# Other SBUF addresses for the tiles of an attention and two-layer MLP kernel

## The chip, the cores and the metric

The kernel runs on one core of a Trainium2 chip. The metric is the device time of one execution in microseconds (us). TensorE is called PE here, VectorE DVE, ScalarE ACT, GpSimd POOL, and the DMA queue of SyncE SP.

## The reference, cut to what matters

Gated linear attention over 4 batches, 8 heads, 768 steps and head dimension 40, then two feed-forward layers over 3072 tokens of 320 features.

```python
for t in range(S):                                  # per batch and head
    m_new = np.maximum(f_gate[:, :, t] + m, i_gate[:, :, t])
    f_stab = np.exp(f_gate[:, :, t] + m - m_new)
    i_stab = np.exp(i_gate[:, :, t] - m_new)
    C = f_stab * C + i_stab * einsum('bhd,bhe->bhde', vt, kt)
    n = f_stab * n + i_stab * kt
    y[:, :, t] = sigmoid(o_gate) * einsum('bhde,bhe->bhd', C, qt) / np.maximum(np.abs(n . qt), 1)
x = y, as [3072, 320]
h = x @ w_in;  x = (np.maximum(h, 0) + alpha * np.minimum(h, 0)) @ w_out      # 320 -> 2048 -> 320
h = max(x @ w1, x @ w2, x @ w3);  out = h @ w_out2                            # 320 -> 768 -> 320
```

All inputs and the output are float32.

## The kernel before, in words

The sequence is cut into 24 chunks of 128 steps (L = 128, 6 chunks for each batch). The chunks are grouped into 7 blocks of 2, 3, 3, 4, 4, 4 and 4 chunks, that is 256, 384 or 512 tokens.

The program has three stretches.

1. **Opening.** Gate tables are computed, attention of the first two chunks runs, and the first layer's weights are loaded. The weights arrive as float32 (`w1_raw`, `wproj_raw`), ACT rounds them to a high part (L710, L714), and DVE or POOL subtract for the low part (L367, L371, L373). `POOL_PIECES` (L125) puts two of these pieces behind `prepare 2` and five behind `prepare 3` in POOL's order, and `prepare 3` waits for `u_bcast` of chunk 3.
2. **Layer 1 of block b beside attention of block b + 1.** `block_plan` (L91) writes the order out by hand: `hidden` (8 matmuls into one PSUM bank, L630) and `project` (8 matmuls, L644 to L649) alternate on PE, and between them stand the attention steps of the next block (scores L556, carry L564 and L571, values L593 to L597, turn L605). ACT and DVE apply the activation and split it into high and low parts (L798, L996, L807, L977). In the last block there is no attention. There the second layer's weights are loaded into the room of the attention tiles and split (L821, L823, L1036, L1040).
3. **Layer 2.** Six blocks of 512 tokens: 18 groups of 8 matmuls (L666) and 6 groups of 12 (L680 to L682) for each, with the maximum taken on DVE (L1017, L1021) and the split on ACT and DVE (L837, L1027). The input `x2_in` comes back from DRAM, alternately into buffers a and b.

Every engine has its own list of instructions in an order fixed when the program is built, and the engines wait for each other by semaphores. All loads and stores go through SP, except three loads on ACT's queue at the start. Loads of a chunk go into one of three slots (`SLOTS`, L61): `q_t` and `k_t` once the state matmuls of three chunks before are done (L392), `kv` once its values are (L402), `u_bcast` once its product is (L408).

SBUF is laid out by hand. `sb(name, shape, dtype)` (L170) gives a tile the bytes at `cursor` of every partition and moves the cursor by the size, rounded up to 32 bytes. With a fourth argument the tile lies at that byte and the cursor stays. The first byte, `base`, is 16,512 (L167 rounds the first free byte, 16,481, up to a multiple of 64). Three rooms are used twice: the second layer's weights and buffer a lie over the attention tiles, buffer b and the gate rows over the tiles of the first layer's tokens, and the second layer's intermediate tiles over `wproj`. The order of use is kept by semaphores. Both layouts use 212,096 bytes of each partition.

The changed lines all stand in this layout part, and the functions that compute are called with the same tiles.

Of the kernel before, what the change touches and what calls it, by code (L numbers as in the profile page):

```python
# [27 lines left out]
F32 = mybir.dt.float32  # L28
F32R = mybir.dt.float32r
# [4 lines left out]
B, H, S, D = 4, 8, 768, 40  # L34
# [9 lines left out]
T = CMAX * L  # L44
DM = H * D
FF1, FF2 = 2048, 768
J1, J2 = FF1 // 128, FF2 // 128
# [6 lines left out]
T2 = 512  # L54
# [8 lines left out]
HID_BANKS, GF_SLOTS, G_SLOTS = 2, 3, 3  # L63
# [95 lines left out]
def build(nc, f_g, i_g, q_t, k_t, kv, o_g, w_in, w_out, alpha, w_max, w_out2, out):  # L159
    with ExitStack() as ctx:  # L160
# [7 lines left out]
        cursor = [base]  # L168

        def sb(name, shape, dt, at=None):  # L170

            size = 4 if dt != BF16 else 2
            for n in shape[1:]:
                size *= n
            offset = cursor[0] if at is None else at
            t = nc.alloc_sbuf_tensor_at(name, shape, dt, offset=offset)
            if at is None:
                cursor[0] += (size + 31) // 32 * 32
            return t, offset


        att_at = cursor[0]
        qt, _ = sb("q_t", [128, SLOTS, NK, L], F32)
        kt, _ = sb("k_t", [128, SLOTS, H, L], F32)
        ub, _ = sb("u_bcast", [128, SLOTS, H, L], F32)
        nat, _ = sb("kv", [128, SLOTS, VO + H * DE], F32)
        og, _ = sb("o_gate", [128, 2, CMAX, DM], F32)
        prob, _ = sb("prob", [128, H, L], F32)
        prob_r, _ = sb("prob_rest", [128, H, L], F32)
        prob_3, _ = sb("prob_3", [128, H, L], BF16)  # L190
        v_parts, _ = sb("v_parts", [128, H, 3, DE], BF16)
        v_r, _ = sb("v_rest", [128, H, D], F32)
        v_w, _ = sb("v_weighted", [128, SLOTS, WG], F32)
        state, _ = sb("state", [128, WG], F32)
        state_dec, _ = sb("state_decayed", [128, H * DE], F32)
        state_new, _ = sb("state_new", [128, NK, KH, DE], F32)
        carried, _ = sb("carried", [128, NK, KH, DE], F32)
        inner, _ = sb("inner", [128, H, DE], F32)
        scale, _ = sb("scale", [128, H, D], F32)
        norm, _ = sb("norm", [128, H], F32)  # L200
        y, _ = sb("y", [128, CMAX, 384], F32)
        tables, _ = sb("tables", [128, 4, NCH, H], F32)
        own, _ = sb("own_rows", [128, NK, KH], F32)
        ident, _ = sb("ident", [128, 128], F32)
        end_at = cursor[0]

        cursor[0] = att_at
        w2h, _ = sb("w2_hi", [128, 3, 3 * FF2], F32R)
        w2l, at = sb("w2_lo", [128, 3, 3 * FF2], F32R)
        w2raw, _ = sb("w2_raw", [128, 3, 3 * FF2], F32, at)  # L210
        wo_h, _ = sb("wout2_hi", [128, J2, DM], F32R)
        wo_l, at = sb("wout2_lo", [128, J2, DM], F32R)
        wo_raw, _ = sb("wout2_raw", [128, J2, DM], F32, at)
        xin_a, _ = sb("x2_in_a", [128, 3, T2], F32)
        x2_a, _ = sb("x2_split_a", [128, 5, T2], F32R)
        cursor[0] = max(end_at, cursor[0])


        xs, _ = sb("x_split", [128, 5, T], F32R)
        gf, gf_at = sb("g_full", [128, GF_SLOTS, T], F32)  # L220
        gh, _ = sb("g_hi", [128, G_SLOTS, T], F32R)
        gl, _ = sb("g_lo", [128, G_SLOTS, T], F32R)
        rows, _ = sb("rows", [128, 3, T], F32)

        gates, _ = sb("gates", [128, 8, S], F32, gf_at)
        assert gf_at + 8 * S * 4 <= cursor[0]

        tokens_end = cursor[0]
        w1h, w1h_at = sb("w1_hi", [128, 3, FF1], F32R)
        w1l, at = sb("w1_lo", [128, 3, FF1], F32R)  # L230
        w1raw, _ = sb("w1_raw", [128, 3, FF1], F32, at)
        wp, wp_at = sb("wproj", [128, J1, 2 * DM], F32R)
        wpraw, _ = sb("wproj_raw", [128, J1, 2 * DM], F32, wp_at)
        alpha_sb, _ = sb("alpha", [128, J1], F32)
        beta, _ = sb("beta", [128, J1], F32)

        end_at = cursor[0]

        cursor[0] = gf_at
        xin_b, _ = sb("x2_in_b", [128, 3, T2], F32)  # L240
        x2_b, _ = sb("x2_split_b", [128, 5, T2], F32R)
        assert cursor[0] <= tokens_end
        cursor[0] = wp_at
        first, _ = sb("first_of_max", [128, 2, T2], F32)
        best, _ = sb("best", [128, 2, T2], F32)
        g2h, _ = sb("g2_hi", [128, 2, T2], F32R)
        g2l, _ = sb("g2_lo", [128, 2, T2], F32R)
        final, _ = sb("final", [128, 2, TT2, DM], F32)
        assert cursor[0] <= wp_at + J1 * 2 * DM * 4
        xin, x2 = [xin_a, xin_b], [x2_a, x2_b]  # L250
        assert end_at <= nc.sbuf_usable_end, (end_at, nc.sbuf_usable_end)

# [939 lines left out]
```

## Time and profile before

| | us |
|---|---|
| median of 3 runs | 786.44 |
| lowest and highest run | 785.37, 786.5 |
| the profiled execution, its own time | 786.5 |
| its span, first to last instruction | 784.7 |

The time of an execution is a little longer than the span that its trace shows: 786.5 against 784.7. A row of the trace gives either one instruction or group, or a sum over a window that is given in us from the start of the span. A PE matmul that is followed by another overlaps with it, so the mean length of one matmul is larger than the distance from one to the next.

### The profile page before, as it was taken

What the parts mean: (1) busy time and instruction counts of PE and PEld (TensorE: products, weight loads), DVE (VectorE), ACT (ScalarE), POOL (GpSimd) and SP (SyncE); (2) the same over time, 40 slices, a digit from 0 to 9 for tenths busy, and PEclk for the clock granted to TensorE, in tenths of its full rate; (3) what the DMA queues carried; (4) which work ended last, traced back from release to release, by engine and by line L of the source; (5) the groups of instructions that cost most, each with busy time, mean ns of one, the idle gap of its engine ahead of it and who ended that gap; (6) DMA issues with size and microseconds to landing.
All of it is one profiled execution on the core that took longest, in us unless ns stands there. A gap on an engine that the chain in (4) does not pass through costs nothing.

```text
span 784.7 us, 11547 instructions
## 1 busy us (share of the span) xinstructions
PE 736.7 (94%) x4410; PEld 653.6 (83%) x4410; DVE 478.2 (61%) x823; ACT 310.1 (40%) x648; POOL 184.3 (23%) x187
## 2 busy tenths in 40 slices
PE   2556999999999999999999999999999999999997
PEld 2545999999998888888888888888888888888886
DVE  6455888878978886888688754934242432434222
ACT  4453455456355444644554345421211212121211
POOL 4266533334525332434233200000000000000000
PEclk9866999999999999999999999999999999999999
DMA  6971232323123221331020054030110202000000
GB/s 195 284 215 53 75 99 78 101 71 114 61 78 107 77 96 43 110 102 65 34 63 0 1 176 130 1 112 2 36 40 0 74 1 74 0 34 1 34 0 34
DMA packets 40057, 56.37 MB, mean 72 GB/s; under 512 B 3457, under 2 KB 29058, under 8 KB 39618
## 3 DMA queue, kind: packets, MB, share of 16 engines
q1 hardware_dynamic: 39570, 54.57, 22.4%
q10 hardware_dynamic: 432, 1.06, 0.4%
q8 instruction: 35, 0.57, 0.3%
q14 instruction: 20, 0.16, 0.1%
HBM read 47.65 MB, written 7.96 MB: 71 GB/s over the span
## 4 chain that ended last, share of the span: by engine, by line
PE 83%; DVE 7%; POOL 3%; DMA 3%; SPq 2%; issue 1%; ACT 1%; ACTq 0%; DVEq 0%; POOLq 0%
PE bank L666 25%; PE bank L630 20%; PE bank L644 5%; PE bank L646 5%; PE bank L645 5%; PE bank L556 4%; PE bank L680 3%; PE bank L681 3%; PE bank L682 3%; PE bank L648 2%; PE bank L649 2%; PE bank L564 1%; PE bank L571 1%; POOL wproj L371 1%; DMA u_bcast<-u_scratch 1%
## 5 line engine op out<-in xcount | busy, mean ns | idle before, releaser
L630 PE MATMUL bank<-x_split,w_hi 128*128 128x512 f32 (+2 forms) x560 | 168.8, 369 | 2.2 <-ACT x_split L762 2.2
L630 PE MATMUL bank<-x_split,w_lo 128*128 128x512 f32 (+2 forms) x336 | 120.9, 362 | 0.0
L630 PEld LDWEIGHTS bank<-x_split,w_hi 128*128 128x128 f32 x560 | 103.6, 191 | 14.9 <-ACT x_split L762 2.6
L798 ACT ACTIVATE g_full<-bank 128x512 f32<-128x512 f32 (+2 forms) x112 | 59.7, 533 | 137.0 <-PE bank L630 136.1
L996 DVE SCALAR_TENSOR_TENSOR g_full<-g_full,beta,bank 128x512 f32<-128x512 f32 (+2 forms) x112 | 74.6, 666 | 34.6 <-ACT g_full L798 34.1
L644 PE MATMUL bank<-g_hi,wproj 128*128 128x512 f32 (+2 forms) x224 | 84.6, 378 | 5.2 <-DVE g_lo L977 5.2
L807 ACT ACTIVATE g_hi<-g_full 128x512 fp32r<-128x512 f32 (+2 forms) x112 | 63.2, 564 | 64.0 <-DVE g_full L996 63.9
L1017 DVE TENSOR_TENSOR best<-bank,first_of_max 128x512 f32<-128x512 f32 x36 | 24.9, 691 | 102.5 <-PE bank L666 76.1
L977 DVE TENSOR_TENSOR g_lo<-g_full,g_hi 128x512 fp32r<-128x512 f32 (+2 forms) x112 | 70.2, 627 | 18.9 <-ACT g_hi L807 18.1
L646 PE MATMUL bank<-g_hi,wproj 128*128 128x512 f32 (+2 forms) x224 | 81.0, 362 | 0.0
L645 PE MATMUL bank<-g_lo,wproj 128*128 128x512 f32 (+2 forms) x224 | 80.8, 361 | 0.0
L837 ACT ACTIVATE g_hi<-best 128x512 fp32r<-128x512 f32 x36 | 22.8, 632 | 128.7 <-DVE best L1021 128.7
L1134 POOL TENSOR_TENSOR prob<-prob_rest 128x512 bf16<-128x512 f32 x44 | 49.1, 1118 | 91.9 <-DVE prob_rest L915 91.9
L666 PE MATMUL bank<-x_split_b,w_hi 128*128 128x512 f32 x270 | 70.4, 390 | 0.0
L666 PE MATMUL bank<-x_split_a,w_hi 128*128 128x512 f32 x270 | 70.4, 390 | 0.0
L630 PEld LDWEIGHTS bank<-x_split,w_lo 128*128 128x128 f32 x336 | 64.3, 191 | 6.8
L772 ACT ACTIVATE u_bcast<-u_bcast,tables 128x128 f32<-128x128 f32 x192 | 59.8, 390 | 8.7 <-POOL u_bcast L1101 8.6
L666 PEld LDWEIGHTS bank<-x_split_a,w_hi 128*128 128x128 f32 x270 | 50.0, 188 | 9.5
L666 PEld LDWEIGHTS bank<-x_split_b,w_hi 128*128 128x128 f32 x270 | 49.9, 188 | 9.4
L556 PE MATMUL bank<-q_t,k_t 120*128 120x128 f32 x384 | 49.8, 285 | 1.7 <-DVE inner L943 1.7
L556 PEld LDWEIGHTS bank<-q_t,k_t 120*128 120x128 f32 x384 | 48.8, 201 | 3.0 <-DVE inner L943 1.9
L644 PEld LDWEIGHTS bank<-g_hi,wproj 128*128 128x128 f32 x224 | 42.7, 190 | 10.3 <-issue 4.6
(115 smaller groups left out, 1399.3 us busy)
## 6 DMA issues: line engine op xcount, KB each, us to landing
u_bcast<-u_scratch SPq DMA_DIRECT2D x24, 512.0 KB, 4.1
kv<-in_kv SPq DMA_DIRECT2D x24, 324.0 KB, 3.0
out<-final SPq DMA_DIRECT2D x6, 640.0 KB, 3.8
q_t<-in_q_t SPq DMA_DIRECT2D x24, 120.0 KB
k_t<-in_k_t SPq DMA_DIRECT2D x48, 60.0 KB
wproj_raw<-in_w_out SPq DMA_DIRECT2D x4, 640.0 KB, 9.9
o_gate<-in_o_gate SPq DMA_DIRECT2D x4, 640.0 KB, 4.9
w_raw<-in_w_max SPq DMA_DIRECT2D x2, 1152.0 KB, 6.3
```

The lines of the kernel that those rows point to most:

```text
L556: ins = pe.matmul(ps[:, k * L:(k + 1) * L], kt[0:KR, c, h, :], qt[0:KR, c, h // KH, :], start=True, stop=True)
L630: ins = pe.matmul(ps[:, 0:cols], w[:, a, f], xs[:, x, 0:cols], start=(m == 0), stop=(m == 7))
L644: pe.matmul(acc[a][:, 0:cols], wa, hi, start=(j == 0), stop=False)
L645: pe.matmul(acc[a][:, 0:cols], wa, lo, start=False, stop=False)
L646: pe.matmul(acc[a][:, 0:cols], wl, hi, start=False, stop=(j == J1 - 1))
L666: ins = pe.matmul(ps[:, :], w[:, a, cols], x2[b2 % 2][:, x, :], start=(k == 0), stop=(k == 7))
L772: ins = act.activation(ub[:, c, h, :], ub[:, c, h, :], ACT.Exp, bias=tables[:, 0, ch, h:h + 1])
L798: act.activation(gf[:, n % GF_SLOTS, 0:cols], hid[j % HID_BANKS][:, 0:cols], ACT.Relu, scale=-1.0).then_inc(neg_done, 1)
L807: act.activation(gh[:, n % G_SLOTS, 0:cols], gf[:, n % GF_SLOTS, 0:cols], ACT.Copy).then_inc(g_hi_done, 1)
L977: dve.tensor_tensor(gl[:, n % G_SLOTS, 0:cols], gf[:, n % GF_SLOTS, 0:cols], gh[:, n % G_SLOTS, 0:cols].bitcast(F32), ALU.subtract).then_i ...
L996: dve.scalar_tensor_tensor(out=g, in0=g, scalar=beta[:, j:j + 1], in1=hid[j % HID_BANKS][:, 0:cols], op0=ALU.mult, op1=ALU.add).then_inc(h ...
L1134: pool.tensor_tensor(prob_3[:, heads, :], prob_r[:, heads, :], high(prob_r[:, heads, :]), ALU.subtract).then_inc(prob_split, 1)
```

## The change: the groups of tiles change places

The diff moves three groups of tiles. No instruction, wait, loop, shape or order is touched. The tiles of a group keep their distances, and the three double uses of a room stay as they were.

| group | tiles | first byte in a partition, before | after | moved by |
|---|---|---|---|---|
| attention, and over it layer 2's weights and buffer a | `q_t` to `ident`, `w2_*`, `wout2_*`, `x2_in_a`, `x2_split_a` | 16,512 | 141,568 | +125,056 |
| tokens, and over them the gate rows and buffer b | `x_split`, `g_full`, `g_hi`, `g_lo`, `rows`, `gates`, `x2_in_b`, `x2_split_b` | 103,552 | 106,752 | +3,200 |
| layer 1's weights, and over `wproj` layer 2's intermediate tiles | `w1_*`, `wproj*`, `alpha`, `beta`, `first_of_max`, `best`, `g2_*`, `final` | 138,368 | 16,512 | -121,856 |

In steps of 256 bytes the first two moves are 488.5 and 12.5 steps, and the third is 476. All three groups started 128 bytes past a multiple of 256 before. After the change the first two start at a multiple of 256, and the third is still 128 bytes past one.

```diff
+        w1h, w1h_at = sb("w1_hi", [128, 3, FF1], F32R)
+        w1l, at = sb("w1_lo", [128, 3, FF1], F32R)
...
+        wp, wp_at = sb("wproj", [128, J1, 2 * DM], F32R)
...
+        xs, _ = sb("x_split", [128, 5, T], F32R)
+        gf, gf_at = sb("g_full", [128, GF_SLOTS, T], F32)
...
+        gates, _ = sb("gates", [128, 8, S], F32, gf_at)
+        assert gf_at + 8 * S * 4 <= cursor[0]
+
         att_at = cursor[0]
         qt, _ = sb("q_t", [128, SLOTS, NK, L], F32)
...
-        xin_a, _ = sb("x2_in_a", [128, 3, T2], F32)
-        x2_a, _ = sb("x2_split_a", [128, 5, T2], F32R)
-        cursor[0] = max(end_at, cursor[0])
-
-
-        xs, _ = sb("x_split", [128, 5, T], F32R)
...
-        tokens_end = cursor[0]
-        w1h, w1h_at = sb("w1_hi", [128, 3, FF1], F32R)
...
-        end_at = cursor[0]
+        end_at = max(end_at, cursor[0])
...
-        assert cursor[0] <= tokens_end
+        assert cursor[0] <= att_at
...
+        cursor[0] = end_at
+        xin_a, _ = sb("x2_in_a", [128, 3, T2], F32, att_at + 4 * (2 * 9 * FF2 + 2 * J2 * DM))
+        x2_a, _ = sb("x2_split_a", [128, 5, T2], F32R, att_at + 4 * (2 * 9 * FF2 + 2 * J2 * DM) + 3 * T2 * 4)
+        end_at = max(end_at, att_at + 4 * (2 * 9 * FF2 + 2 * J2 * DM) + 8 * T2 * 4)
```

## Rows read from the trace of the kernel before

**Rows 1.** The page's first part: busy time, share, instructions of each engine.

```profile
PE 736.7 (94%) x4410; PEld 653.6 (83%) x4410; DVE 478.2 (61%) x823; ACT 310.1 (40%) x648; POOL 184.3 (23%) x187
```

**Rows 2.** Windows (start:end, length, busy us, granted clock, DMA share, GB/s).

```profile
17.00:50.00 33.00, 15.59 (x96) 14.30 (x96) 13.97 (x34) 17.73 (x40) 12.30 (x11) 0.75 1.03 288
50.00:110.00 60.00, 49.91 (x418) 48.44 (x418) 45.52 (x88) 25.64 (x68) 37.74 (x32) 0.86 0.22 73
110.00:518.00 408.00, 407.83 (x2584) 362.82 (x2583) 317.98 (x556) 204.84 (x428) 126.99 (x127) 1.00 0.24 75
518.00:780.00 262.00, 261.15 (x1301) 225.97 (x1299) 89.31 (x124) 52.94 (x97) 0.00 (x0) 1.00 0.10 31
```

**Rows 3.** Waits of PE from 110 us on (total us, times, longest).

```profile
PE bank L680 <- DVE g_lo L1027: 0.4, 1, 0.4
PE bank L593 <- DVE carried L923: 0.2, 1, 0.2
```

**Rows 4.** The chain that ended last, opening (start us, us, what).

```profile
40.56 9.42 DMA u_bcast<-u_scratch
...
50.16 1.05 POOL u_bcast L1101
51.22 0.70 POOL v_weighted L1094
51.92 2.32 POOL w_lo L367
...
67.32 1.01 POOL prob L1134
...
70.45 1.89 PE bank L630 x8
...
74.05 1.07 PE bank L630 x8
...
78.00 0.91 PE bank L556 x8
```

**Rows 5.** POOL's wait for the DMA, whole span (total us, times, longest).

```profile
POOL u_bcast L1101 <- DMA u_bcast<-u_scratch: 28.7, 4, 11.0
```

**Rows 6.** Groups by form, 462 to 510 us (count, busy us, mean ns, idle).

```profile
L630 PEld LDWEIGHTS bank<-x_split,w_hi 128*128 128x128 f32 x71 | 13.3, 188 | 2.8
L645 PEld LDWEIGHTS bank<-g_lo,wproj 128*128 128x128 f32 x25 | 4.7, 188 | 1.0
...
L630 PE MATMUL bank<-x_split,w_lo 128*128 128x512 f32 x43 | 16.7, 389 | 0.0
L645 PE MATMUL bank<-g_lo,wproj 128*128 128x512 f32 x24 | 9.3, 389 | 0.0
```

**Rows 7.** Groups by form, 560 to 770 us.

```profile
L666 PE MATMUL bank<-x_split_b,w_lo 128*128 128x512 f32 x153 | 43.0, 389 | 0.0
L666 PE MATMUL bank<-x_split_a,w_lo 128*128 128x512 f32 x108 | 30.3, 389 | 0.0
...
L666 PEld LDWEIGHTS bank<-x_split_a,w_hi 128*128 128x128 f32 x180 | 33.3, 188 | 6.3
```

**Rows 8.** Groups by form on POOL, 17 to 70 us.

```profile
L371 POOL TENSOR_TENSOR wproj<-wproj_raw,wproj 128x1024 fp32r<-128x1024 f32 x4 | 9.6, 2401 | 0.0
L367 POOL TENSOR_TENSOR w_lo<-w_raw,w_hi 128x1024 fp32r<-128x1024 f32 x3 | 7.0, 2347 | 0.0
L1101 POOL TENSOR_SCALAR_AFFINE_SELECT u_bcast<-u_bcast 128x1024 f32<-128x1024 f32 x4 | 4.8, 1208 | 28.7 <-DMA u_bcast<-u_scratch 28.7
L1094 POOL TENSOR_TENSOR v_weighted<-kv,tables 128x328 f32<-128x328 f32 x4 | 2.9, 734 | 0.0
```

**Rows 9.** DMA issues, 80 to 400 us (count, KB each, median us to landing).

```profile
u_bcast<-u_scratch SPq DMA_DIRECT2D x18, 512.0 KB, 4.1
kv<-in_kv SPq DMA_DIRECT2D x18, 324.0 KB, 2.9
o_gate<-in_o_gate SPq DMA_DIRECT2D x4, 640.0 KB, 4.9
```

**Rows 10.** Landing of the 18 kv loads, then the 18 u_bcast loads.

```profile
DMA to landing us min/median/max: 2.7/2.9/3.8
DMA to landing us min/median/max: 3.7/4.1/5.6
```

**Rows 11.** DMA part of the trace, 17 to 50 us.

```profile
DMA packets 6649, 9.49 MB, mean 288 GB/s; under 512 B 515, under 2 KB 5248, under 8 KB 6647
```

**Rows 12.** Windows at the clock's step, columns as in rows 2.

```profile
61.00:70.00 9.00, 3.58 (x28) 3.21 (x29) 1.73 (x4) 3.25 (x7) 9.00 (x8) 0.50 0.00 0
70.00:74.00 4.00, 4.00 (x25) 4.00 (x22) 3.82 (x10) 2.04 (x7) 0.01 (x1) 0.50 0.62 210
75.00:78.00 3.00, 3.00 (x27) 3.00 (x27) 1.92 (x5) 1.62 (x5) 2.02 (x2) 1.00 0.01 4
```

More of the change, by code:

```diff
@@ L179, in sb @@
             return t, offset
+        w1h, w1h_at = sb("w1_hi", [128, 3, FF1], F32R)
+        w1l, at = sb("w1_lo", [128, 3, FF1], F32R)
+        w1raw, _ = sb("w1_raw", [128, 3, FF1], F32, at)
+        wp, wp_at = sb("wproj", [128, J1, 2 * DM], F32R)
+        wpraw, _ = sb("wproj_raw", [128, J1, 2 * DM], F32, wp_at)
+        alpha_sb, _ = sb("alpha", [128, J1], F32)
+        beta, _ = sb("beta", [128, J1], F32)
+        xs, _ = sb("x_split", [128, 5, T], F32R)
+        gf, gf_at = sb("g_full", [128, GF_SLOTS, T], F32)
+        gh, _ = sb("g_hi", [128, G_SLOTS, T], F32R)
+        gl, _ = sb("g_lo", [128, G_SLOTS, T], F32R)
+        rows, _ = sb("rows", [128, 3, T], F32)
+        gates, _ = sb("gates", [128, 8, S], F32, gf_at)
+        assert gf_at + 8 * S * 4 <= cursor[0]
         att_at = cursor[0]
@@ L213, in build @@
         wo_raw, _ = sb("wout2_raw", [128, J2, DM], F32, at)
-        xin_a, _ = sb("x2_in_a", [128, 3, T2], F32)
-        x2_a, _ = sb("x2_split_a", [128, 5, T2], F32R)
-        cursor[0] = max(end_at, cursor[0])
-        xs, _ = sb("x_split", [128, 5, T], F32R)
[L220 to L226, printed above, removed]
-        tokens_end = cursor[0]
-        w1h, w1h_at = sb("w1_hi", [128, 3, FF1], F32R)
[L230 to L235, printed above, removed]
-        end_at = cursor[0]
+        end_at = max(end_at, cursor[0])
         cursor[0] = gf_at
```

## The prediction

> **What bounds the kernel now.** I read the busy table first, then a cut of the span into windows, then PE's waits, and last the chain of waits in the window that was left.
>
> The busy table names PE: 736.7 of 784.7 us [rows 1]. The windows say where the rest is. From 110 to 518 us PE is busy for 407.83 of 408.00 us, and from 518 to 780 us for 261.15 of 262.00 us, at a granted clock of 1.00, the 2.4 GHz level [rows 2]. The list of PE's waits from 110 us on has two entries, 0.4 and 0.2 us [rows 3]. So from 110 us to the last matmul at about 779 us the end is set by how fast PE goes through a fixed list, and by nothing else. What DVE, ACT, POOL or a DMA gain or lose there stays hidden until it is large enough to make PE wait.
>
> The first 110 us are different. From 17 to 50 us the DMA share is 1.03, so the transfers fill their engines [rows 2]. The chain goes through the load of `u_bcast` for chunk 3, issued at 40.56 us and landed 9.42 us later. From there it goes through POOL's serial work (mask, weighting, then low parts of weights) to 68.3 us and then to PE [rows 4]. POOL waits 28.7 us for `u_bcast` loads over the whole span, in four waits [rows 5], and all of it falls before 70 us [rows 8].
>
> **The change, part by part.** It adds no instruction, removes none, moves none in any queue and adds no wait. Its cost can lie only in the length of existing instructions and transfers at other addresses. So the question for each kind is whether a row shows its length to depend on the address.
>
> *PE's matmuls and weight loads, first layer.* The weights `w1_hi` to `wproj` lie from byte 138,368 on, `w2_*` from 16,512 on. After the change they have nearly swapped rooms. Loading 128x128 weights takes 188 ns from `w1_hi`, 188 ns from `wproj` [rows 6] and 188 ns from `w2_hi` [rows 7]. The three rooms span nearly all of what is used. The matmul with 512 columns takes 389 ns for `x_split` (from 103,552), 389 ns for `g_lo` (from 126,080) [rows 6], 389 ns for `x2_split_b` (from 119,936) and 389 ns for `x2_split_a` (from 93,312) [rows 7]. A difference of 1 ns would have shown. The cost is 0: equal to the ns at both ends of the memory. As bounds I take half of the last digit, 0.5 of 389 ns, which is 0.13%. Over the 669 us from 110 to 779 us that would be +0.9 or -0.9 us, and I hold it for very unlikely that the rounding hides all of it.
>
> *ACT, DVE and POOL on moved tiles.* On POOL the subtraction of 1024 elements takes 2401 ns at `wproj` and 2347 ns at `w1`, that is 2.3 ns for each element. 328 elements in the attention room take 734 ns, 2.2 ns each [rows 8]. These rooms lie some 140,000 bytes apart, the same engine works on them at the same pace, and these rooms swap. Value taken: 0. The bound comes from the 54 ns between the two 1024-element rows, 2.3%. On the chain POOL has 18.2 us between 50.16 and 68.33 us [rows 4], so 0.4 us in either direction. After 110 us the same operations are off the path, where 2.3% of POOL's 127 us over 408 us can't become the bound [rows 2].
>
> *DMA into moved tiles.* This is where something in the addresses does change: the rows of attention and token tiles now start at a multiple of 256 bytes instead of 128 past one. In the trace no load has such a start, so its effect isn't shown directly. The nearest rows are loads with other starts. The three `kv` slots of 2,592 bytes start 128, 160 and 192 bytes past a multiple of 256, and a row of `o_gate` 224 past one. From `kv` (324 KB, 2.9 us) to `u_bcast` (512 KB, start 128, 4.1 us) the landing grows by 1.2 us for 188 KB, 6.4 ns for each KB. From there to `o_gate` (640 KB, start 224, short pieces of 1,280 bytes) it grows by 0.8 us for 128 KB, 6.3 ns for each KB [rows 9]. A load with the worst start lies on the line of the others, so I take 0 for this part as well.
>
> For bounds I take the spread among equal loads. `kv` lands in 2.7 at best against 2.9 us in the median (7%), `u_bcast` in 3.7 against 4.1 us (10%) [rows 10]. From 17 to 50 us 9.49 MB move [rows 11]. Into moved tiles with a new start go three chunks of 512 + 324 + 320 KB, one `o_gate` of 480 KB and a table of 96 KB, together 4.04 MB, 43%. 7% of 43% of 33 us is 1.0 us, and 10% is 1.4 us. A gain there would be passed on in full: the chain waits for that load [rows 4], and the POOL and PE work behind it is serial up to 110 us. The upper end is +1.4 us, since nothing shown excludes a slower start. The loads of weights (5.1 MB) move by a whole number of 256-byte steps. Loads after 110 us end nowhere near PE's path [rows 3]. The last store, out of `final`, keeps its start too.
>
> The Trainium skill has a rule on this, on the page "DMA: Bandwidth & Descriptors", section "How a descriptor splits into AXI transactions". A descriptor that doesn't start at a 256-byte boundary has a first transaction that begins at the boundary below, and the bytes in front still cost time. By that count a 512-byte row at start 128 takes 20 beats and an aligned one 16, and a 4,096-byte row 132 against 128. An estimate from the page's figures is 20% on 0.96 MB of `q_t` and `k_t` rows and 3% on the other 3.1 MB, 0.29 of 9.49 MB, about -1.0 us. By that rule `o_gate` at start 224 should lie above the line, and the rows don't bear that out. It is the first rival below.
>
> **The sum.** 784.7 us of span + 0 (PE) + 0 (ACT, DVE, POOL) + 0 (DMA) = 784.7 us, and 1.8 us lie around the span, which gives 786.5 us. That is 0.06 us above the median of the runs. I forecast **786.4 us**, the median. A difference below 0.2%, 1.6 us, counts as no change, since the runs of the kernel before alone lie 1.1 us apart.
>
> **The rivals.**
>
> 1. *Aligned starts shorten the loads.* For it: the opening is bound by DMA and 43% of its bytes change their start. Against it: start 224 costs nothing visible. Price: -1.0 us by the working above, 785.4 us, and at most -1.4 us. Even in this case the result is mostly below what can be told from no change.
> 2. *The clock's step in the opening falls later.* This is the one on the other side. The granted clock is 0.50 (1.2 GHz) from 61 to 74 us, where PE has only 3.58 us of work in the first 9 us, and 1.00 from 75 us on, with PE busy without a gap from 70 us [rows 12]. A group of eight L630 matmuls takes 1.89 us at the low level and 1.07 us at the high one [rows 4]. If a shift of about 1 us in the opening's transfers makes the rise miss this point, the 3.95 us of work from 74.05 to 78.00 us take 3.95 x 1.89 / 1.07 = 7.0 us. The chain runs on PE there and nothing gives it back: +3.0 us, 789.4 us. It decides from the point at which the rise comes after about 76 us. Against it: no part of the sum moves the opening by more than a fraction of a us, and three runs show no such jump.
> 3. *An engine's access depends on the address in a way that these rows miss.* Attention's small tiles were only ever seen in the lower half. A general 0.3% on PE's attention and layer work is 2 us, which gives 784.4 or 788.4 us. For it speaks only that each small tile has one address in the trace. Against it stand four groups of equal PE rows and POOL's equal pace.
>
> **How the numbers follow.** No change that matters: 0.78. Rival 1: 0.11, of which 0.03 falls beyond 0.2%. Rival 2: 0.04. Rival 3: 0.07, half to each side. Faster by more than 0.2%: 0.03 + 0.035 and 0.015 for drift of the measurement, 0.08. Slower: 0.04 + 0.035, with 0.005 for drift, 0.08. Within: 0.84. The range reaches from rival 1's far end with some drift, 786.4 - 1.6 = 784.8 us, to the bound of the DMA part above, 786.4 + 1.4 + 0.2 of drift = 788.0 us. It leaves out rival 2 and the outer parts of rival 3.
>
> **What would show it.** The windows 110 to 518 and 518 to 780 us again have PE busy for more than 99.5%, the 512-column matmul again takes 389 ns and the weight load 188 ns. `wproj` on POOL again takes about 2.4 us, and `kv`, `u_bcast` and `o_gate` land in 2.9, 4.1 and 4.9 us. The PE clock again rises near 74 us. Rival 1 would show as shorter landings of `kv` and `u_bcast` (2.7 and 3.7 in the median) and the POOL chain starting near 49 us. Rival 2 would show a clock of 0.50 in 75 to 78 us. The prediction is wrong if a PE row of the same shape changes by more than 1 ns, or if PE gets waits after 110 us that it didn't have.

## The result and the profile after

| | before | after |
|---|---|---|
| median, us (6 runs each) | 786.03 | 791.58 |
| lowest to highest | 785.37 to 787.22 | 790.06 to 792.39 |
| span of the profiled execution | 784.7 | 788.7 |

The ratio is 1.0066, with a 95% interval of 1.0053 to 1.0080. The changed layout is 5.5 us slower, and the profiled execution (790.44 us) is one of its quick ones.

The line numbers of the changed kernel are 2 lower from the compute part on (L630 is L628 there, L666 is L664). The windows of the changed kernel answer to [rows 2] and have the same columns.

```profile
17.00:50.00 33.00, 16.62 (x99) 15.31 (x99) 14.07 (x34) 17.72 (x40) 13.47 (x13) 0.71 1.04 297
50.00:110.00 60.00, 50.25 (x425) 49.10 (x426) 45.25 (x87) 26.68 (x71) 36.60 (x31) 0.87 0.20 67
110.00:518.00 408.00, 407.93 (x2557) 359.80 (x2556) 317.32 (x554) 202.98 (x424) 126.92 (x127) 1.00 0.23 75
518.00:780.00 262.00, 262.00 (x1298) 226.51 (x1297) 89.55 (x125) 52.57 (x95) 0.00 (x0) 1.00 0.10 31
780.00:788.00 8.00, 3.14 (x20) 2.61 (x18) 0.77 (x2) 2.06 (x5) 0.00 (x0) 1.00 0.23 82
```

PE is as full as before and its clock is as high, but in the window of 408 us it gets through 2557 matmuls instead of 2584. So it doesn't wait longer, it steps more slowly. The list of PE's waits from 110 us on has become shorter than [rows 3]:

```profile
PE bank L678 <- DVE g_lo L1025: 0.4, 1, 0.4
```

The chain of waits shows the step. First the kernel before, in its last block of layer 1 and at the start of layer 2:

```profile
508.14 1.81 PE bank L630 x8
...
511.76 1.81 PE bank L630 x8
...
519.02 10.88 PE bank L666 x48
```

The same two groups, the last `hidden` ones of layer 1, in the changed kernel:

```profile
511.36 1.86 PE bank L628 x8
...
515.08 1.87 PE bank L628 x8
...
522.52 10.89 PE bank L664 x48
```

Eight matmuls take 1.86 or 1.87 instead of 1.81 us, and from one group of eight `hidden` matmuls to the next it is 3.72 instead of 3.62 us. The changed kernel comes to the first of these groups 3.2 us later than the kernel before and ends layer 1 3.5 us later, though it was 1.7 us ahead at the first scores of block 1 (110.28 against 112.02 us). Layer 2 runs at 10.89 against 10.88 us for 48 matmuls, nearly unchanged. The groups by form, 462 to 510 us, answer to [rows 6]:

```profile
L628 PE MATMUL bank<-x_split,w_lo 128*128 128x512 f32 x42 | 16.6, 394 | 0.0
...
L643 PE MATMUL bank<-g_lo,wproj 128*128 128x512 f32 x24 | 9.5, 394 | 0.0
...
L628 PEld LDWEIGHTS bank<-x_split,w_hi 128*128 128x128 f32 x70 | 13.2, 188 | 3.1
```

Those from 560 to 770 us answer to [rows 7]:

```profile
L664 PE MATMUL bank<-x_split_b,w_lo 128*128 128x512 f32 x150 | 42.3, 390 | 0.0
...
L664 PE MATMUL bank<-x_split_a,w_lo 128*128 128x512 f32 x114 | 32.1, 390 | 0.0
```

The load of weights still shows 188 ns. It is the matmul that went from 389 to 394 ns, in layer 1 alone. A better measure is the distance from the start of one matmul to the start of the next, as an average over some 500 neighbours with 512 columns that follow each other without a gap between 380 and 519 us. It is 227.5 ns before and 232.4 ns after. For 384 columns (110 to 230 us) it is 174.3 and 176.0 ns, and for layer 2's matmuls with 320 columns 146.2 and 147.3 ns.

By the trace layer 1 from the first scores of block 1 on (112.0 to 519.0 us before, 110.3 to 522.5 us after) is 5.2 us longer and layer 2 0.5 us. Together that is 5.7 us, the whole difference of the medians (5.5 us) within their uncertainty. By blocks, each from its first `hidden` matmul to that of the next: the two with 384 columns take 0.5 and 0.3 us more (58.0 and 63.0 us before), the three with 512 columns and attention beside them 1.0 us each (76.4 to 76.5 us before), and the last, without attention, 1.4 us (58.1 us before).

**What the slow matmuls share.** PE reads two tiles in a matmul, the weights and the moving columns. The table has their starting addresses modulo 256.

| pair | before | after | distance of matmuls |
|---|---|---|---|
| `w1_*` and `x_split`, `wproj` and `g_*` (layer 1) | 128 and 128 | 128 and 0 | +4.9 ns at 512 columns |
| `w2_*` and `x2_split_a`, `x2_split_b` (L666) | 128 and 128 | 0 and 0 | none |
| `g2_*` and `wout2_*` (L680 to L682) | 128 and 128 | 128 and 0 | +1.1 ns at 320 columns, as an average within a group of 12 |

In the kernel before the two starts agree in every one of these pairs. The change moved the groups by distances that are whole steps of 256 for one of them and half steps for the others.

The third row is not a steady cost like the first. In a group of 12 the distance behind the first matmul grows from 143.4 to 154.3 ns and that behind the second from 145.0 to 150.0 ns, the fourth falls from 146.0 to 140.0 ns, and the rest alternate between about 148.4 and 145.0 ns, on average as before. A whole group takes 1.765 instead of 1.755 us.

### The profile page after: what moved, and what is told of

The parts are those of the page before. It is cut to its first block, busy times and chain, and to the rows that moved or that the text cites. A ratio compares the mean times of both kernels' runs of the same rounds, so it can differ in the third digit from the quotient of the medians.

```text
span 788.7 us, 11547 instructions
## 1 busy us (share of the span) xinstructions
PE 742.5 (94%) x4410; PEld 655.7 (83%) x4410; DVE 478.6 (61%) x823; ACT 309.9 (39%) x648; POOL 184.6 (23%) x187
## 4 chain that ended last, share of the span: by engine, by line
PE 83%; DVE 7%; DMA 3%; POOL 3%; issue 1%; ACT 1%; SPq 1%; ACTq 0%; DVEq 0%; POOLq 0%
PE bank L664 25%; PE bank L628 20%; PE bank L642 5%; PE bank L643 5%; PE bank L644 5%; PE bank L554 4%; PE bank L678 3%; PE bank L679 3%; PE bank L680 3%; PE bank L646 3%; PE bank L647 3%; PE bank L562 1%; PE bank L569 1%; POOL wproj L369 1%; PE bank L591 1%
## 5 line engine op out<-in xcount | busy, mean ns | idle before, releaser
L628 PE MATMUL bank<-x_split,w_hi 128*128 128x512 f32 (+2 forms) x560 | 170.6, 372 | 2.2 <-ACT x_split L760 2.2
L628 PE MATMUL bank<-x_split,w_lo 128*128 128x512 f32 (+2 forms) x336 | 122.0, 365 | 0.0
L628 PEld LDWEIGHTS bank<-x_split,w_hi 128*128 128x128 f32 x560 | 103.8, 191 | 15.9 <-ACT x_split L760 2.6
L796 ACT ACTIVATE g_full<-bank 128x512 f32<-128x512 f32 (+2 forms) x112 | 59.7, 533 | 143.4 <-PE bank L628 141.7
L1015 DVE TENSOR_TENSOR best<-bank,first_of_max 128x512 f32<-128x512 f32 x36 | 24.9, 692 | 102.8 <-PE bank L664 76.4
L628 PEld LDWEIGHTS bank<-x_split,w_lo 128*128 128x128 f32 x336 | 64.4, 192 | 7.4
L664 PE MATMUL bank<-x_split_b,w_hi 128*128 128x512 f32 x270 | 70.3, 390 | 0.0
L664 PE MATMUL bank<-x_split_a,w_hi 128*128 128x512 f32 x270 | 70.3, 390 | 0.0
L664 PEld LDWEIGHTS bank<-x_split_a,w_hi 128*128 128x128 f32 x270 | 50.0, 188 | 9.5
L664 PEld LDWEIGHTS bank<-x_split_b,w_hi 128*128 128x128 f32 x270 | 49.9, 188 | 9.3
```

What stands on the lines that cost most here:

```text
L628: ins = pe.matmul(ps[:, 0:cols], w[:, a, f], xs[:, x, 0:cols], start=(m == 0), stop=(m == 7))
L664: ins = pe.matmul(ps[:, :], w[:, a, cols], x2[b2 % 2][:, x, :], start=(k == 0), stop=(k == 7))
L796: act.activation(gf[:, n % GF_SLOTS, 0:cols], hid[j % HID_BANKS][:, 0:cols], ACT.Relu, scale=-1.0).then_inc(neg_done, 1)
```

## The experiments

All are compared with runs of the kernel before on the same chip. "Start" means the address modulo 256.

**Which relation matters.** Four layouts, with these edits:

```diff
# e1: the changed kernel
+        cursor[0] += 128
         xs, _ = sb("x_split", [128, 5, T], F32R)
# e2: the kernel before
+        cursor[0] += 128
         w1h, w1h_at = sb("w1_hi", [128, 3, FF1], F32R)
# e3: the kernel before
+        cursor[0] += 128
         xs, _ = sb("x_split", [128, 5, T], F32R)
# e4: the changed kernel
+        cursor[0] += 64
         xs, _ = sb("x_split", [128, 5, T], F32R)
```

e1: 

> The changed layout with 128 free bytes put ahead of the token tiles, so that tokens and attention start 128 bytes past a multiple of 256 again and the first layer's weights (also 128 past) keep their place below them. In the trace of the changed kernel the distance from one 512-column matmul of layer 1 to the next grew from about 227 to 232 ns (the mean length of one from 389 to 395 ns). Theory A (the two operands that PE reads, weights and moving columns, slow each other when their addresses differ by 128 modulo 256): back to 389 ns in layer 1, and about 785 to 786 us. Theory B (the moving tile may not start at a multiple of 256, whatever the weights do): also 389 ns. Theory C (the weights lie in a worse room, below the tokens): still 395 ns and about 791 us.

e2: 

> The kernel before with 128 free bytes ahead of the first layer's weights alone: rooms in the order of before, attention and tokens at their old addresses, weights at a multiple of 256. Theory A (difference of the two operands modulo 256): 395 ns for the 512-column matmul of layer 1, 389 ns for L666, about 0.4 ns more for L680 to L682, and 786 + 6.5 + 0.5 = about 792 to 793 us. Theory B (start of the moving tile): 389 ns everywhere and 786 us. Theory C (room of the weights): 389 ns and 786 us.

e3: 

> The kernel before with 128 free bytes ahead of the token tiles: tokens and first-layer weights both start at a multiple of 256, attention and the second layer's weights stay 128 past one, buffer b of layer 2 moves with the tokens. Theory A (difference of the two operands): 389 ns in layer 1, 389 ns for L666 on buffer a, 395 ns for L666 on buffer b (432 matmuls by 5.5 ns, +2.4 us), and the L680 group 0.5 us longer, about 789 us. Theory B (start of the moving tile): 395 ns in layer 1 and on buffer b, about 795 us. Theory C: 389 ns everywhere, 786 us.

e4: 

> The changed layout with 64 free bytes ahead of the token tiles: the first layer's weights and their moving tiles now differ by 64 modulo 256 (128 in the changed kernel, 0 before). Theory A has no curve yet: if only the exact 128 hurts, 389 ns and 786 us; if the cost depends on the difference steadily, something near 392 ns and 788 to 789 us; if any difference but 0 costs the same, 395 ns and 791 us. Theory C (room of the weights): 395 ns.

| | starts of attention, tokens, weights | median, us | ratio to before, interval | 512 columns, layer 1 |
|---|---|---|---|---|
| e1 | 128, 128, 128 | 785.66 | 0.9998 (0.9988 to 1.0009) | 227.4 ns |
| e2 | 128, 128, 0 | 791.14 | 1.0066 (1.0047 to 1.0085) | 232.3 ns |
| e3 | 128, 0, 0 | 787.02 | 1.0018 (1.0007 to 1.0029) | 227.6 ns |
| e4 | 64, 64, 128 | 791.33 | 1.0072 (1.0057 to 1.0087) | 233.3 ns |

The groups by form from 462 to 510 us, first of e1:

```profile
L629 PE MATMUL bank<-x_split,w_hi 128*128 128x512 f32 x71 | 23.1, 389 | 0.0
```

then of e2:

```profile
L631 PE MATMUL bank<-x_split,w_hi 128*128 128x512 f32 x67 | 22.2, 395 | 0.0
```

e1 keeps the changed order of rooms and has the pace of before, so the room of the weights (theory C) is not the cause. e2 keeps the order of before, moves only the weights by 128 bytes, and has the pace of the changed kernel. Its moving tiles haven't moved at all, so theory B falls too. The time is 1 to 2 us below what the expectation added up. e3 has the most to show in one trace. Tokens and first-layer weights moved together and are at pace in layer 1. In layer 2 buffer b, which moved with the tokens, now differs by 128 from `w2`, and buffer a doesn't. Groups by form of e3, 560 to 770 us:

```profile
L667 PE MATMUL bank<-x_split_a,w_lo 128*128 128x512 f32 x108 | 30.5, 390 | 0.0
L667 PE MATMUL bank<-x_split_b,w_lo 128*128 128x512 f32 x153 | 44.0, 395 | 0.0
```

The same instruction with the same weights is slower on every other block of tokens, by the start of its moving tile. At 512 columns theory A holds in e1, e2 and e3, and e4 doesn't go against it. The pace term of e3 is 2.3 us in the trace of layer 2 (268.2 against 265.9 us), but the median rose by only 1.1 us, to 787.0 instead of the expected 789 us. The rest is taken up below.

At 320 columns theory A as it stands is not enough. In e3 `g2_*` and `wout2_*` differ by 128 throughout, yet a group of 12 takes 1.765 us in the blocks of buffer a and 1.755 us, the time of before, in the blocks of buffer b. What differs is the work ahead of it, the L667 groups at pace in the first case and slow in the second. So the small cost at 320 columns depends on what ran before and not on the pair's own starts alone, and it stays unexplained.

e4's expectation left three forms open. The groups by form of e4, 462 to 510 us:

```profile
L629 PE MATMUL bank<-x_split,w_hi 128*128 128x512 f32 x69 | 22.8, 394 | 0.0
L629 PE MATMUL bank<-x_split,w_lo 128*128 128x512 f32 x41 | 16.3, 398 | 0.0
```

A difference of 64 costs at least as much as one of 128 at 512 columns. The distance between 384-column matmuls doesn't grow (174.2 ns against 174.3), where 128 costs 1.7 ns. So the cost depends on the number of columns as well. In e4's trace 0.7 us is something else: PE waits 0.9 us once for DVE's `carried` (L592), where the kernel before waits 0.2 us [rows 3].

**A smaller difference, and which of two matmuls pays.**

```diff
# e7: the kernel before
+        cursor[0] += 32
         w1h, w1h_at = sb("w1_hi", [128, 3, FF1], F32R)
# e8: the kernel before
+        cursor[0] += 128
         w1l, at = sb("w1_lo", [128, 3, FF1], F32R)
         w1raw, _ = sb("w1_raw", [128, 3, FF1], F32, at)
+        cursor[0] += 128
         wp, wp_at = sb("wproj", [128, J1, 2 * DM], F32R)
```

e7: 

> The kernel before with the first layer's weights moved up by 32 bytes alone, so that they differ from their moving tiles by 32 modulo 256. A difference of 128 cost 5 ns for each 512-column matmul and 2 ns for each with 384 columns, one of 64 the other way cost 6 and 0 ns. If only the position in a 64-byte step counts as a match, 32 costs about as much as 64 (395 ns for 512 columns); if the cost grows with the difference, 390 to 392 ns; if a difference below 64 is harmless, 389 ns and 786 us.

e8: 

> The kernel before with only the low part of w_in moved by 128 bytes; w_hi, wproj and all other tiles keep the same start modulo 256. Theory A1 (a matmul suffers from the address of its own weights): the 192 matmuls x_split,w_lo with 512 columns are 5 ns further from their successor and those of w_hi are as before. Theory A2 (the load of the next weights runs beside the stream of the columns, and these two reads disturb each other): the matmul ahead of each w_lo, three of the five w_hi in a group of eight, is 5 ns longer, and that of w_lo is as before. Either way about 3 of 8 L630 matmuls pay, some +1.5 us in total.

e7 took 792.26 us (one run), with 233.2 ns at 512 columns and 173.9 ns at 384. Already 32 bytes cost the full amount, so there is no steady growth and no harmless step of 64.

e8 took 789.68 us (one run). The timeline of PE in e8 has one group of eight `hidden` matmuls and the start of the `project` group behind it (start us, us, ...):

```profile
492.77 0.40 PE L632 MATMUL bank<-x_split,w_hi 128*128 128x512 f32 x1
493.00 0.40 PE L632 MATMUL bank<-x_split,w_lo 128*128 128x512 f32 x1
493.24 0.40 PE L632 MATMUL bank<-x_split,w_hi 128*128 128x512 f32 x1
493.47 0.40 PE L632 MATMUL bank<-x_split,w_lo 128*128 128x512 f32 x1
493.70 0.85 PE L632 MATMUL bank<-x_split,w_hi 128*128 128x512 f32 x3
494.39 0.40 PE L632 MATMUL bank<-x_split,w_lo 128*128 128x512 f32 x1
494.63 0.39 PE L646 MATMUL bank<-g_hi,wproj 128*128 128x512 f32 x1
...
496.44 0.40 PE L632 MATMUL bank<-x_split,w_hi 128*128 128x512 f32 x1
```

The `hidden` group takes 1.86 us and the `project` group, whose tiles agree, 1.81 us. Averaged over 29 such groups, with gaps over 260 ns left out, the eight distances are 232.5 (hi), 232.8 (lo), 233.5 (hi), 233.6 (lo), 227.6 (hi), 228.1 (hi), 232.9 (hi) and 234.8 ns (lo). The places of lo are slow, and so is each place just ahead of one. Only the two that neither use nor precede a `w_lo` are at pace. Each of A1 and A2 expected one of the two sets, and the run shows both. So in this group a matmul is slowed if its own weights or the next ones differ from its columns, and once both differ, as in the changed kernel, it isn't slowed twice. Another reading fits e8 alone just as well and wasn't tested by itself: the six slow places are also those where the next weights have another start than the matmul's own. It can't be the only rule, since in e2 all the layer's weights start alike and all 512-column matmuls are slow. Why this is so stays open.

The price in e8's expectation, 1.5 us, was too low. Six of eight matmuls pay instead of three, and its trace has layer 1 2.6 us longer than before (409.6 against 407.0 us). Its single time stands 4.2 us above the median of before, and the rest is not explained.

**The opening.** The profiled execution of the changed kernel was 1.7 us ahead at 110 us. Whether aligned loads do that was tried with these:

```diff
# e5: the kernel before; e9 to e12 start from it
-        base = (nc.sbuf_base + 63) // 64 * 64
+        base = (nc.sbuf_base + 63) // 64 * 64 + 128
# e6: the changed kernel, the same line and
+        cursor[0] += 128
         xs, _ = sb("x_split", [128, 5, T], F32R)
# e9: e5 and
+        cursor[0] += 128
         xs, _ = sb("x_split", [128, 5, T], F32R)
# e10: e5 and 128 bytes ahead of q_t and ahead of u_bcast
# e11: e5 and 128 bytes ahead of u_bcast and ahead of kv
# e12: e5 and kv slots of 2,816 bytes, 96 bytes behind o_gate
```

e5: 

> The kernel before with every tile moved up by 128 bytes: rooms and distances as before, all three groups at a multiple of 256. In the changed kernel the opening was about 1.7 us shorter than before (first 16 score matmuls of block 1 at 110.3 us instead of 112.0), in the three experiments with attention at 128 past a multiple it was 0.1 to 0.5 us shorter. Theory A for the pace: 389 ns for 512-column matmuls in both layers. For the opening, theory D (loads into aligned rows are shorter): these matmuls at about 110.3 us again, and 784.5 us. Theory E (the opening just varies from execution to execution): anywhere from 110 to 112 us, and a median of 786 us.

e6: 

> The changed order of rooms with all three groups at a multiple of 256. Theory A: 389 ns in layer 1, no +5.5 us. Theory D (aligned loads): about 784.5 us, faster than both kernels. Theory E: 786 us. Theory C (room of the weights): 791 us.

e9: 

> The order of rooms of before; attention (and layer 2's weights and buffer a over it) at a multiple of 256, tokens and the first layer's weights 128 past one as before. In six traces with attention 128 past a multiple the first 16 score matmuls of block 1 came at 110.9 to 112.6 us (mean 111.8), in three with it at a multiple at 109.0 to 110.6 us (mean 110.0); the token tiles at a multiple alone (e3) left it at 111.6. Theory D (loads into attention tiles are shorter when their rows start at a multiple of 256): about 110 us here. Theory E (chance, or another group's start): 111.8 us. Theory A: 389 ns in layer 1, and again about 392 to 395 ns for L666 on buffer b alone (+2.3 us), with the L680 group +0.5 us. Total by D and A: 785.5 - 1.8 + 2.8 = 786.5 us; by E and A: 788.3 us.

e10: 

> As e5 (everything at a multiple of 256, 783.5 us against 785.5 us for before), but q_t and k_t 128 bytes past one again. Their loads are made of 512-byte pieces, the shortest of the large ones. If the gain of e5 sits in these, the 2 us are lost again: 785.5 us, score matmuls of block 1 at about 111.8 us. If not, 783.5 us and about 110 us.

e11: 

> As e5, but u_bcast 128 bytes past a multiple of 256 again. Its rows of 4096 bytes would lose only a small part to a ragged start: if the cost is by the piece, 783.5 to 783.8 us and about 110 us for the score matmuls of block 1. If the load that the chain waits for must itself be aligned, 785.5 us and about 111.8 us.

e12: 

> As e5, with 224 bytes of padding in each kv slot and 96 behind o_gate, so that all three kv slots and o_gate start at a multiple of 256 too (they started 0, 32, 64 and 96 past one). If aligned starts shorten loads in general, another 0.2 to 0.6 us in the opening, about 783.1 us; if only the q_t and k_t pieces matter, 783.5 us.

| | starts of attention, tokens, weights | median, us | ratio to before, interval |
|---|---|---|---|
| e5 | 0, 0, 0 | 783.47 | 0.9976 (0.9966 to 0.9986) |
| e6, changed order of rooms | 0, 0, 0 | 784.04 | 0.9980 (0.9969 to 0.9990) |
| e9 | 0, 128, 128 | 788.38 | 1.0028 (1.0016 to 1.0041) |
| e10, `q_t`, `k_t` at 128 | 0, 0, 0 | 785.02 | 0.9987 (0.9976 to 0.9999) |
| e11, `u_bcast` at 128 | 0, 0, 0 | 783.64 | 0.9972 (0.9961 to 0.9982) |
| e12 | 0, 0, 0 | 783.65 | 0.9973 (0.9963 to 0.9983) |

The last load that POOL waits for and POOL's first work after it, in e9:

```profile
41.46 9.72 DMA u_bcast<-u_scratch
...
51.36 1.05 POOL u_bcast L1102
```

and in e5:

```profile
40.02 9.03 DMA u_bcast<-u_scratch
...
49.22 1.06 POOL u_bcast L1101
```

From this POOL instruction to the first scores of block 1 it is 61.0 to 61.9 us in all fourteen traces (the two kernels and twelve experiments), while the instruction itself starts between 47.6 us (e6) and 51.4 us (e9). So most of what moves the opening lies ahead of it, in when this load is issued and when it lands. One trace varies too much to price a layout: e10's has one of the earliest starts (47.9 us), and its median is not among the lowest.

e9 also repeats the test of e3 with the other group moved. Its tokens have the old start, `w2` has the new one, and again buffer b alone is slow (groups by form, 560 to 770 us):

```profile
L667 PE MATMUL bank<-x_split_a,w_lo 128*128 128x512 f32 x109 | 30.9, 390 | 0.0
L667 PE MATMUL bank<-x_split_b,w_lo 128*128 128x512 f32 x150 | 43.1, 395 | 0.0
```

For the gain of the opening the median's change, less what the trace shows from the first scores of block 1 to the end of the span (672.7 us before), is more telling than the opening of a single trace. That leaves -0.2 us for the changed kernel (0, 0, 128), -0.2 for e1 (128, 128, 128), -0.4 for e2 (128, 128, 0), -0.2 for e9 (0, 128, 128), -1.4 for e3 (128, 0, 0), -1.8 for e5 and -1.2 for e6 (0, 0, 0). The intervals of the ratios make each of these uncertain by 0.8 to 1.5 us, e2 the most.

e9 goes against theory D in the form in which it was put: attention's tiles alone bring nothing. e5, e6, e11 and e12 go against theory E: four layouts are faster than the kernel before, clear of 1 in their intervals. As far as these uncertainties allow, the gain appears where tokens and first-layer weights both start at 0. e11 says that `u_bcast` isn't part of it, and e12 that aligned slots of `kv` add nothing. e10 is 1.4 us behind e11, with intervals that overlap, so `q_t` and `k_t` may be part of it. But half of that may have another reason, for e10's trace has a wait of PE behind the opening that was 0.2 us in e11's and in the kernel before:

```profile
PE bank L595 <- DVE carried L925: 0.9, 1, 0.9
```

By the same working as above e10 comes to -1.5 us, e11 to -2.1 and e12 to -2.2. The transfer that carries the gain was not found.

## Why the prediction was wrong, point by point

- **What bounds the kernel** was right, and it is what made the change dear. From 110 us on PE is busy for 407.93 of 408.00 us, so what its matmuls lose goes into the time. An estimate from the distances, 1,024 matmuls with 512 columns at 4.9 ns and 512 with 384 columns at 1.7 ns, is 5.9 us, and layer 1 grew by 5.2 us. The difference lies in the blocks with attention beside them (1.0 us each, where 256 matmuls would make 1.3 us), and its reason is open.
- **The step that failed** is the first of the sum, "PE's matmuls and weight loads, first layer", with its "cost is 0". It took the equal 389 ns of four moving tiles and the equal 188 ns of three rooms of weights as proof that the address doesn't matter. All these rows had one thing in common: the weights and the columns had the same start modulo 256. Among its matmuls with 320 or more columns the trace of before had no pair with another relation (attention's `q_t` and `state`, at 128 columns, start 64 bytes apart, before and after alike), so it said nothing about the one property that the change altered for PE. The bound of half a digit, 0.9 us, was taken from rows that couldn't bound it. In place of 0 the trace shows 5.2 us in layer 1 (389 to 394 ns in the rows, 227.5 to 232.4 ns from start to start) and 0.5 us in layer 2. e2 shows it most plainly: 128 bytes of padding, 5.2 us.
- The section on the change had the numbers below its table: moves of 488.5, 12.5 and 476 steps, the last one downwards. They were held against the starts of DMA rows only, and not against each other for the two reads of one matmul.
- **Rival 3** (an engine's access depends on the address in a way that the rows miss) was the case that came, with a chance of 0.07, half of it for slower, and a size of 2 us. It was priced as a vague 0.3%. The size was 5.5 us, 2.2% of the distance of layer 1's matmuls with 512 columns.
- **ACT, DVE and POOL at 0** held. Groups by form on POOL, 17 to 70 us, changed kernel [rows 8]:

```profile
L369 POOL TENSOR_TENSOR wproj<-wproj_raw,wproj 128x1024 fp32r<-128x1024 f32 x4 | 9.6, 2407 | 0.0
L365 POOL TENSOR_TENSOR w_lo<-w_raw,w_hi 128x1024 fp32r<-128x1024 f32 x3 | 7.0, 2349 | 0.0
```

- **DMA at 0** held for the changed kernel. Landing of the `kv` and the `u_bcast` loads in it, 80 to 400 us [rows 10]:

```profile
DMA to landing us min/median/max: 2.7/3.0/3.8
DMA to landing us min/median/max: 3.7/4.1/5.8
```

  Rival 1 (aligned starts) brought nothing that can be told here, -0.2 us of the median. With all three groups aligned the remainder is -1.2 to -1.8 us, about the size priced. But with attention alone aligned there is none to be seen (e9), though that is where the loads that the rival counted go, so the agreement in size is luck as far as the runs show.
- **Rival 2** (the clock's step falls later) didn't happen. The clock rose inside the window 70 to 74 us, earlier than in [rows 12]:

```profile
70.00:74.00 4.00, 4.00 (x28) 4.00 (x28) 3.83 (x12) 2.86 (x9) 0.00 (x0) 0.76 0.64 218
```

- **What would show it wrong** was put rightly: a PE row of the same shape that changes by more than 1 ns.

## What to carry to other kernels

When a change touches only addresses, list for each instruction all the operands it reads at once and how their starts relate modulo a power of two, and ask which of these relations occur in the trace at all. Rows that agree prove nothing about a relation that they all share. In a kernel bound by PE like this one, with float32r operands and 512 columns, try the same start modulo 256 for weights and moving tiles. Here padding of 128 bytes was worth 5 us, and moving everything to a multiple of 256 made the kernel 0.24% faster than it was (e5).

## What the runs showed of the hardware

- A float32r matmul with 512 columns is 4.9 ns (128 bytes), 5.8 ns (64) or 5.7 ns (32) further from the next if weights and columns differ by that much modulo 256 (e2, e4, e7; 32 bytes in one run), and not at all if they differ by whole steps of 256 bytes (e1, e3, e5, e6). With 384 columns it is 1.7 ns at 128 and nothing at 64 and 32.
- With 320 columns and a difference of 128 a group of 12 takes 1.765 instead of 1.755 us behind 512-column groups at pace, and 1.755 us behind slow ones (e3, e9).
- The length that the profile gives for the weight load, 188 ns, doesn't show it.
- The Trainium skill, page "SBUF — State Buffer", section "Who interferes with whom", gives PE two independent read ports, one for the moving operand and one for the weights, and says that PE never waits on anyone. For the two reads of PE itself the runs don't agree with independent ports: with all instructions unchanged, 128 bytes between the starts decide over 2% of the pace at 512 columns (e2 against before, 232.3 against 227.5 ns). The measurement decides. That the ports are where it arises is not shown.
